# Turn of the next block's inputs, one weight cast, two weight loads and six products put in another order in a two-part expert kernel

## What is computed

```
B, S, D, E, F = (2, 768, 512, 8, 1024)
logits = np.einsum('bsd,de->bse', x, w_gate)
...
            e = fresh_e or prev_e            # by the token's local gate
...
            h = np.maximum(x[b, s] @ w1[e], 0.0)
            out[b, s] = p[e] * (h @ w2[e])
```

## Time and profile before

| | |
|---|---|
| median of 3 runs | 425.1 us (423.46 to 425.39) |
| profiled execution, its own time | 423.02 us |
| its span, first to last instruction | 420.5 us |
| granted TensorE clock, mean | 0.997 |
| PE busy | 406.0 us |
| expert stage, from about | 200 us to the end |

### The profile page before, as it was taken

How to read it: one execution, slowest core, us unless ns; L and a number is a source line. 1 busy time by engine, 2 the same in 40 slices (tenths; PEclk the granted TensorE clock), 3 DMA queues, 4 the chain that set the end, 5 groups by cost and what they waited for, 6 DMA issues and landing times.

```text
span 420.5 us, 7363 instructions
## 1 busy us (share of the span) xinstructions
PE 406.0 (97%) x2637; PEld 333.1 (79%) x2638; DVE 238.8 (57%) x309; ACT 211.0 (50%) x293; POOL 100.7 (24%) x104
## 2 busy tenths in 40 slices
PE   7999999999999999999999999999989999999992
PEld 3888799887889987778787778787667878777782
DVE  4888749982004977686277622118773274663761
ACT  2344678670115764561557432338763284755661
POOL 3354782000000000027621412221122222031220
PEclk9999999999999999999999999999999999999998
DMA  8999900000520009555474932225786367493720
GB/s 292 408 410 416 383 1 2 0 2 0 200 101 0 2 0 389 211 202 163 130 287 149 400 129 94 75 100 203 299 311 244 100 235 307 128 399 127 258 87 4
DMA packets 28442, 76.16 MB, mean 181 GB/s; under 512 B 4927, under 2 KB 14399, under 8 KB 24064
## 3 DMA queue, kind: packets, MB, share of 16 engines
q1 hardware_dynamic: 25216, 67.26, 42.1%
q0 software_dynamic: 2912, 8.13, 5.8%
q10 hardware_dynamic: 288, 0.41, 0.3%
HBM read 62.68 MB, written 14.42 MB: 183 GB/s over the span
## 4 chain that ended last, share of the span: by engine, by line
PE 84%; ACT 7%; issue 3%; ACTq 1%; DMA 1%; DVE 1%; POOL 0%; DVEq 0%; POOLq 0%
PE ps L1039 23%; PE ps L1043 22%; PE ps L1040 22%; ACT wx L616 4%; PE ps L1312 4%; PE ps L1071 3%; PE ps L1092 3%; PE ps L1089 2%; PE ps L1055 1%; PE ps L1138 1%; DMA kv<-qkv 1%; ACT os L681 1%; DVE xF L957 1%; ACT hs L664 1%; ACT hT L674 1%
## 5 line engine op out<-in xcount | busy, mean ns | idle before, releaser
L970 DVE TENSOR_TENSOR hT<-ps,hT 128x512 fp32r<-128x512 f32 x34 | 23.5, 692 | 83.5 <-ACT hT L674 83.5
L951 DVE TENSOR_TENSOR wx<-raw_w,wx 128x1024 fp32r<-128x1024 f32 x56 | 65.1, 1220 | 2.8 <-ACT wx L616 2.8
L1039 PE MATMUL ps<-wx,hT 128*128 128x512 f32 x136 | 55.7, 409 | 0.3
L616 ACT CAST wx<-raw_w 128x1024 fp32r<-128x1024 f32 x56 | 55.0, 1046 | 0.0
L1043 PE MATMUL ps<-wx,hT 128*128 128x512 f32 x136 | 54.8, 403 | 0.0
L1043 PE MATMUL ps<-wx,xT 128*128 128x512 f32 x136 | 54.5, 401 | 0.0
L1039 PE MATMUL ps<-wx,xT 128*128 128x512 f32 x136 | 53.5, 393 | 0.0
L1040 PE MATMUL ps<-wx,hT 128*128 128x512 f32 x136 | 53.3, 392 | 0.0
L1040 PE MATMUL ps<-wx,xT 128*128 128x512 f32 x136 | 53.2, 391 | 0.0
L494 POOL DMA_INDIRECT out<-os,snow x16 | 18.8, 1176 | 104.9 <-ACT os L681 104.9
L1039 PE MATMUL ps<-x,win 128*128 128x384 f32 x128 | 43.2, 337 | 0.0
(11 more groups left out here) (165 smaller groups left out, 726.4 us busy)
## 6 DMA issues: line engine op xcount, KB each, us to landing
raw_w<-w_exp SPq DMA_DIRECT2D x28, 1024.0 KB, 7.1
qk<-qkv SPq DMA_DIRECT2D x7, 768.0 KB, 9.5
raw_first<-w_exp SPq DMA_DIRECT2D x4, 1024.0 KB, 7.7
x_block<-xg SPq DMA_DIRECT2D x16, 256.0 KB, 2.0
xq<-x_block SPq DMA_DIRECT2D x64, 64.0 KB
kv<-qkv SPq DMA_DIRECT2D x4, 768.0 KB, 11.2
x_rows<-x2n SPq DMA_DIRECT2D x11, 256.0 KB, 2.8
kv<-qkv SPq DMA_DIRECT2D x7, 384.0 KB, 10.0
```

What stands on the lines that cost most here:

```text
L616: nc.scalar.copy(wx[:, slot, 0, c], raw).then_inc(wx_hi[w], 1)
L951: nc.vector.tensor_tensor(wx[:, slot, 1, c], raw, wx[:, slot, 0, c].bitcast(F32), ALU.subtract).then_inc(w2_lo_dve if w else w1_lo_dve, 1)
L970: nc.vector.tensor_tensor(lo, psHT[:, 512 * a:512 * a + 512], hi.bitcast(F32), ALU.subtract).then_inc(hT_done, 1)
L1039: mm(o, lh, rl, start=first, stop=False)
```

## The change

It has four parts.

1. DVE: `turn_x(g + 1)` stands between `h_lo(g, 0)` and `h_lo(g, 1)` in `step`, and behind `h_lo(g, 0)`, ahead of the weight piece 3, in `first_step`.
2. ACT, in `first_step` alone: `relu(g, 0)` stands ahead of `evac_before`, and weight piece 3 behind `h_hi(g, 0)`.
3. SP, once, at the border of the stages: the two halves of `raw_w2` are issued together, ahead of the store of the second column half, and the wait for `gathered` at 32 is gone, so that the two transfers of `raw_w1[0]` are issued as soon as `x2_done` is complete.
4. PE, once: in `first_w1` the products stand in the order (0,0), (0,1), (1,0), (2,0), (3,0), (1,1), (2,1), (3,1) of (k, a), `last_rows` behind the first, and `turn_h(0, 0)` behind (1,1).

```diff
@@ SP @@
                 if n == 0:
                     sp.wait_ge(gathered, 16)
-                    raw(1, 1, raw_w2, raw_w2_in, (0,))
+                    raw(1, 1, raw_w2, raw_w2_in)
             sp.wait_ge(x2_done, TT + 1)
-            sp.wait_ge(gathered, 32)
-            raw(1, 1, raw_w2, raw_w2_in, (1,))
             raw(0, 2, raw_w1[0], raw_w1_in[0])
@@ ACT @@
             def first_step(g, e, slot):
 
+                relu(g, 0)
                 evac_before(g, o_done)
-                relu(g, 0)
+                h_hi(g, 0)
                 if e is not None:
                     weights_hi(0, e, slot, (3,))
-                h_hi(g, 0)
                 relu(g, 1)
                 h_hi(g, 1)
@@ DVE @@
             def step(g):
 
                 h_lo(g, 0)
+                turn_x(g + 1, 64 * g)
                 h_lo(g, 1)
+                x_lo(g + 1, xF[:].rearrange("p k t -> p (k t)"))
+
+            def first_step(g, e, slot):
+
+                h_lo(g, 0)
                 turn_x(g + 1, 64 * g)
-                x_lo(g + 1, xF[:].rearrange("p k t -> p (k t)"))
-
-            def first_step(g, e, slot):
-
-                h_lo(g, 0)
                 if e is not None:
                     weights_lo(0, e, slot, (3,))
                 h_lo(g, 1)
-                turn_x(g + 1, 64 * g)
                 x_lo(g + 1, xF[:].rearrange("p k t -> p (k t)"))
@@ PE @@
-                for k, a in ((0, 0), (0, 1), (1, 0), (1, 1), (2, 0), (3, 0), (2, 1), (3, 1)):
-                    if (k, a) == (1, 0):
+                for k, a in ((0, 0), (0, 1), (1, 0), (2, 0), (3, 0), (1, 1), (2, 1), (3, 1)):
+                    if (k, a) == (0, 1):
                         last_rows(TT - 1, TT + 1, (2, 3))
...
-                    if (k, a) == (2, 1):
+                    if (k, a) == (1, 1):
                         turn_h(0, 0)
```

## The result

The changed kernel takes 429.69 us in the median of 4 runs (428.31 to 431.65), the kernel before beside it 424.9 us. The ratio is 1.0127, with a 95% interval of 1.01 to 1.0154: slower by 4.2 to 6.5 us. The median is past the end of the range, 429.0. The profiled execution took 429.32 us with a span of 426.8, where the earlier trace rows are of a span of 420.5.

The account below looks back on a forecast made before the run. PE, busy 406.0 of 420.5 us, was taken as the bound, with 7.0 us to win in the expert stage. Gather wait +2.1, borders' gains and late `xq` summed to +0.9 us (bounds -1, +4): 426.0 us, range 421.5 to 429.

Parts of the forecast that it names:

- ACT's wait: At the border b7 to b8: ACT's wait of 1.38 us for the turned inputs goes.
- the chain of transfers behind b9's wait: From b8's gather to b9's `xq`: no engine there gets faster, so all behind the gather's landing moves by 0.7 us.
- the zero of PE's order: In `first_w1`: the new order of products costs zero, hidden by PE's own work; uncovered 0.2 us either way.
- Landing about 208.9: PE waits 2.1 us: Border of the stages: block 1's gather, issued at 204.3, lands late beside 2 MB of loads; bounds 0.7 and 5.3 us.
- The estimate that the prediction took from the Trainium skill, 208.3: Border of the stages: with queues taking turns, block 1's gather lands about 4 us after issue; PE waits 1.4 us.
- b9 leaves +2.4: In b9: the second low part waits for `xq` and ends at 326.3 instead of 323.87; b9 leaves 2.4 us later.
- PE has no slack there: In b9: PE's part k=4 follows at the end of `h_lo(9, 1)`, so a late `xq` is paid in full.
- Taken together b8 comes 2.2 us nearer: Border b7 to b8: b8's transposes come 2.2 us nearer to b7's, bounds 1.4 and 2.98.
- Behind b9 the borders give back 2.1: From b10 to b16: the borders of experts become 2.1 us shorter in all.
- +0.3 each: In b3, b12 and b14: `xq` comes late and costs 0.3 us in each.
- The slow side: Border of the stages: gather pays 7.95 us or loads hold the store; PE waits 5.0, end 428.9; chance 0.17.
- if gather, store and `xq` between 302 and 321 come in time with PE: Rival for b9: transfers follow PE, so b9 doesn't wait; sum -4.4 us, end 420.7; chance 0.15.

Follow-up runs that it names:

- w2_early: The changed kernel with the wait for block 1's gather back ahead of the loads of raw_w1[0] alone; 1.0070 of the kernel before.
- warm_fill: The changed kernel with 15 products of zeros added behind first_w1, ahead of the wait for block 1's gather; 1.0100 of the kernel before.
- quarter loads: Both kernels with a quarter of the bytes in the expert loops' weight loads, output not the reference's; kernel before 0.9966, changed kernel 0.9959.
- turn_only: The kernel before with DVE's part of the change alone; 0.9994 of the kernel before.
- act_only: The kernel before with ACT's part of the change alone; 0.9995 of the kernel before.
- sp_old: The changed kernel with SP's part undone, the parts of DVE, ACT and PE kept; 1.0047 of the kernel before.
- act_first_turn: The kernel before with ACT's part, and the early turn in the first block of each expert alone; 0.9947 of the kernel before.
- pe_only: The kernel before with PE's order in first_w1 alone; 0.9994 of the kernel before.
- gather_first: The kernel before with the gather issued ahead of the scatter in POOL's step; 0.9980 of the kernel before.

## Why the prediction was wrong

**Mechanisms.** ACT's wait, the two places of PE's new waits, the chain of transfers behind b9's wait and the zero of PE's order came out as written. The sum, +0.9 us, was wrong; it measured +4.8 in the medians and +6.3 between the two profiled executions. Counted where they arise, these 5.4 us between forecast and profiles are: 1.2 more wait at the border of the stages, 1.6 lower clock behind it, 0.3 less up to b7, 1.4 more in the chain of transfers from b7 to b9, 1.6 more behind b9's wait from the lower clock, 0.1 less behind b10. The terms of the prediction:

- *"Landing about 208.9: PE waits 2.1 us".* It landed at 210.2 and PE waited 3.24. The gather was issued at 205.06, not 204.3: the store's data came 2 us later behind the loads, not 1.2. And the loads beside it cost 1.8 us, not 1.3. w2_early divided the two. The estimate that the prediction took from the Trainium skill, 208.3, was farther off still: the gather landed only when the transfers had drained (share 0.08 from 209 to 210).
- *No term for the clock.* This is the step that failed: 3.2 of the 5.4 us stand there. The prediction counted an idle PE by its idle time alone. At the border the turn comes 3.32 us later and 1.56 more are lost to the clock; together they are b1's delay of 4.88, and warm_fill shows that the second goes when PE isn't idle. In b9 a like stretch at 0.5 follows the wait; its 1.8 us, of which about 0.3 fall on a slack that PE had there, are worked out from the rows, not tried. How much of the border's part reaches the end is open: warm_fill, without it, ended 0.4 us earlier in the spans and 0.8 in the medians. The Trainium skill, "TensorE: Matmul & The Clock Gate", Part 1, says that an idle engine falls back to 1.2 GHz and is given 2.4 GHz again only after sustained work. The rows of 210 to 215 agree: the grant fell behind an idle stretch of 3.24 us and came back after 3.4 us of work. Nothing in the rows ahead of the prediction showed it, since PE's longest wait in the expert stage of the kernel before was 2.29 us and the grant stayed at 1.00 there.
- *"b9 leaves +2.4".* This term is mis-sized: the second low part ended at 330.2 instead of 323.87, +6.3. The chain was right, its start was not: the prediction had b7 at +0.9, it was at +3.4, with the border's two misses. `x_block` of b8 follows at 305.79 (+3.7), the next weights at 309.86 (+3.7), and their load held the store 2.5 us longer than before, `xq` +4.8. With the clock b10 is +7.9. "PE has no slack there" was nearly right: about 0.3 us.
- *"Taken together b8 comes 2.2 us nearer"*: 1.68. The gap between casts and `relu` counted as issue was 0.75 us, not 0.27.
- *"Behind b9 the borders give back 2.1"* and *"+0.3 each"* for b3, b12 and b14: 1.64 came back. DVE did wait for `xq` in these three, 1.26 to 1.56 us, and PE didn't. It also waited 1.07 us in b8, where the prediction had no wait.
- *The slow side* had nearly the right end, 428.9, by luck. Its sign, a gather landing behind 210.5, was not met (210.2); the end came from a smaller wait, the clock, and b9. *"if gather, store and `xq` between 302 and 321 come in time with PE"*, the fast rival, is what the quarter loads make true: with them the experts' stage gives 5.1 us.

**The gap of 0.75 us.** The chain names what ACT's queue does in it: it reads the next expert's block range (`value_load`, lines 322 and 323). From its pieces behind the sixth of the seven casts:

```profile
305.94 0.27 ACTq L322
...
306.55 0.54 ACTq L323
...
307.43 0.06 ACT hs L662
```

The casts end at 306.68, the reading at 307.32. In the kernel before it ended at 304.90, 0.04 us behind the casts.

**The parts don't add.** Alone they measure +1.04%, -0.06, -0.05 and -0.06; together +1.27, and the three without SP's +0.47. turn_only and act_only each won 1.5 to 2 us at the borders and each lost it again where transfers were late, in b1 or between b8 and b10. Together, in sp_old, they wait longer in both places (2.05 and 3.72 us against 1.85 and 2.29 in turn_only), and the clock fell behind both waits. b7 comes 2.3 us later there than in the kernel before, and so do the gather behind it (296.88 and 294.18) and `xq` of b9 (323.23 and 320.76).

**Open.** Why the reading of the block range took longer isn't shown. Nor is what decides the clock's fall at the shorter waits: 2.29 us in b8 left it at 1.00 in the kernel before and 2.38 in act_first_turn, while it fell behind 2.30 in pe_only, 2.29 in turn_only and 1.96 in act_only. It isn't fixed for a kernel either: in 26 runs of the kernel before, beside gather_first, the mean grant goes from 0.989 to 0.997. The eight runs at 0.990 or below took 423.8 to 424.8 us, the eight at 0.996 or above 422.9 to 424.3. So it can be a part of the spread of 2 us, not all of it, and one profile tells only of its own execution.

## What to carry to other kernels

Where loads, gathers and small stores share the transfer engines, follow the chain of transfers through their issues before an engine's order is changed: engines that get ahead of it wait at it, and a wait put in front of a tight consumer is then paid in full. A wait on a semaphore that seems to hold a load back for nothing may be what keeps the small, urgent transfer fast. Issuing the small one first was worth 1.1% here where its lateness was paid for (sp_old), and 0.2% where it wasn't. A wait of TensorE can have a second price behind it: look at the granted clock after each new one, in more than one execution.

## What was not expected of the hardware

An idle TensorE of 3.24 us was followed by 3.4 us at half the clock, worth 1.6 us; filling it with products of zeros kept the clock at 1.00. Behind waits of 4.2 to 4.4 us in b9 the same cost 1.8 us where the grant fell after PE was back (the changed kernel), and 3.0 where it fell during the wait (w2_early). The store of 128 KB in small pieces landed 4.17 us after its issue between 2 MB of loads ahead of it and 2 MB behind, where it landed within 3 us with the transfers idle. A gather of 256 KB took 3.3 to 3.5 us alone, 5.1 us beside 2 MB, 7.8 us (311.57 to 319.32) beside 4 MB.
